# The last stage of an attention and experts kernel takes the tokens without an expert first, and prepares its first group in the experts' last tile

## What is computed

```python
NT, D, E, F = 3072, 512, 8, 1024          # 4 batches x 768 tokens
# experts
do_compute = (x @ w_skip) > 0             # the other tokens keep their x
e_idx = argmax(x @ w_gate)                # one expert for each computed token
gate_w = softmax(x @ w_gate)[e_idx]
x[mask] = x[mask] + gate_w * (relu(x[mask] @ w1[e]) @ w2[e])   # w1[e] 512x1024, w2[e] 1024x512
# last stage
h = maximum(maximum(x @ w1, x @ w2), x @ w3)                   # 512x768 each
out = h @ w_out                                                # 768x512
```

## Time and profile before

| | us |
|---|---|
| median of 3 runs | 704.7 (704.05 to 705.7) |
| profiled execution | 703.12, its span 701.3 |
| PE busy | 663.9 (95%) |
| DVE busy | 468.5 (67%) |
| ACT busy | 326.8 (47%) |
| POOL busy | 125.6 (18%) |
| mean granted clock of PE | 0.985 of full speed |

### The profile page before, as it was taken

One profiled execution on the slowest core, in us unless ns is written; L12 is line 12 of the kernel. 1 busy time (PEld: TensorE's weight loads), 2 busy tenths in 40 slices (PEclk: granted clock), 3 DMA queues, 4 the chain that ended last, 5 costly groups with the idle time before them and its releaser, 6 DMA issues.

```text
span 701.3 us, 13203 instructions
## 1 busy us (share of the span) xinstructions
PE 663.9 (95%) x4903; PEld 555.2 (79%) x4903; DVE 468.5 (67%) x811; ACT 326.8 (47%) x509; POOL 125.6 (18%) x153
## 2 busy tenths in 40 slices
PE   4999965999999999996899999999999999999998
PEld 3778852899999999984688888878888887888886
DVE  4778867666567656757898886258878625887510
ACT  3445422555555555545455645244554525455321
POOL 7321122425444545440000000000000000000000
PEclk9999986999999999999999999999999999999999
DMA  8999954655765565566111111511111111110011
GB/s 301 411 335 325 363 193 176 231 196 194 236 221 194 184 229 202 189 219 233 37 60 61 60 36 71 179 46 61 60 62 32 73 61 45 61 61 30 1 54 67
DMA packets 34548, 102.57 MB, mean 146 GB/s; under 512 B 5644, under 2 KB 5772, under 8 KB 34384
## 3 DMA queue, kind: packets, MB, share of 16 engines
q1 hardware_dynamic: 30640, 96.04, 39.2%
q0 software_dynamic: 3296, 5.00, 2.0%
q10 hardware_dynamic: 576, 1.05, 0.4%
HBM read 89.20 MB, written 16.79 MB: 151 GB/s over the span
## 4 chain that ended last, share of the span: by engine, by line
PE 52%; DMA 2%; DVE 2%; ACT 1%; issue 1%; POOL 0%; SPq 0%; DVEq 0%; POOLq 0%; ACTq 0%
PE ps_c L1333 8%; PE ps_c L1334 8%; PE ps_c L1335 8%; PE ps_b L1333 5%; PE ps_b L1335 5%; PE ps_b L1334 5%; PE ps_f L1334 2%; PE ps_f L1333 2%; PE ps_f L1335 2%; PE ps_a L1333 2%; PE ps_a L1335 2%; PE ps_a L1334 2%; DMA x_in<-x_dram,idx_g 1%; DMA f_in<-x_dram 1%; PE ps_a L1395 0%
## 5 line engine op out<-in xcount | busy, mean ns | idle before, releaser
L991 DVE TENSOR_TENSOR w_lo<-raw,w_hi 128x1024 fp32r<-128x1024 f32 x66 | 82.4, 1258 | 52.6 <-ACT w_hi L650 52.6
L650 ACT ACTIVATE w_hi<-raw 128x1024 fp32r<-128x1024 f32 x67 | 71.0, 1059 | 61.1 <-PE ps_y L1335 50.5
L1333 PE MATMUL ps_c<-c_hi,u_lo 128*128 128x512 f32 x216 | 85.8, 397 | 4.9 <-DVE c_lo L1061 2.9
L1014 DVE TENSOR_TENSOR u_lo<-u_f,u_hi 128x1792 fp32r<-128x1792 f32 x27 | 54.7, 2025 | 52.0 <-ACT u_hi L640 48.1
L1334 PE MATMUL ps_c<-c_lo,u_hi 128*128 128x512 f32 x216 | 84.2, 390 | 0.0
L1335 PE MATMUL ps_c<-c_hi,u_hi 128*128 128x512 f32 x216 | 84.1, 389 | 0.0
L1333 PE MATMUL ps_h<-x_hi,w_lo 128*128 128x256 f32 x256 | 72.3, 283 | 0.6 <-DVE x_lo L998 0.3
L1335 PE MATMUL ps_h<-x_hi,w_hi 128*128 128x256 f32 x256 | 72.4, 283 | 0.0
L1334 PE MATMUL ps_h<-x_lo,w_hi 128*128 128x256 f32 x256 | 72.4, 283 | 0.0
L609 ACT ACTIVATE f_u<-ps_c 128x512 f32<-128x512 f32 x58 | 34.7, 598 | 67.5 <-PE ps_c L1335 65.2
L640 ACT ACTIVATE u_hi<-u_f 128x1792 fp32r<-128x1792 f32 x27 | 46.0, 1702 | 29.4 <-PE ps_c L1335 27.6
(11 more groups left out here) (217 smaller groups left out, 1453.4 us busy)
## 6 DMA issues: line engine op xcount, KB each, us to landing
raw<-wpack SPq DMA_DIRECT2D x67, 512.0 KB, 3.9
u_f<-wunit SPq DMA_DIRECT2D x27, 512.0 KB, 3.3
v_sb<-vW SPq DMA_DIRECT2D x32, 390.0 KB, 5.7
k_sb<-kT SPq DMA_DIRECT2D x32, 250.0 KB, 5.1
q_sb<-qT SPq DMA_DIRECT2D x16, 384.0 KB, 6.1
x_dram<-x_buf SPq DMA_DIRECT2D x4, 1536.0 KB, 10.5
out<-f_out SPq DMA_DIRECT2D x24, 256.0 KB, 2.0
f_in<-x_dram SPq DMA_DIRECT2D x2, 2048.0 KB, 9.1
```

The costliest lines, as they stand in the source:

```text
L650: act.activation(w_hi[c % RING][:, :], raw[:, c % RAW, :], ACT.Copy).then_inc(s_whi, 1)
L991: dve.tensor_tensor(w_lo[c % RING][:, :], raw[:, c % RAW, :], w_hi[c % RING][:, :].bitcast(F32), ALU.subtract).then_inc(s_wlo, 1)
L1014: dve.tensor_tensor(u_lo[n % UBUF][:, 1:8, :], u_f[n % UBUF][:, 1:8, :], u_hi[n % 2][:, :, :].bitcast(F32), ALU.subtract).then_inc(s_ulo, 1)
L1333: pe.matmul(out_, a_lo, b_hi, start=first, stop=False, skip_group_check=goes_on)
```

## The change

**Order of tokens.** The last stage takes its 3072 tokens in an order of its own: first those without an expert, then the rest. DVE works out each token's place from the ranks (a ninth column in the one-hot rows counts the tokens without an expert). POOL writes the token numbers to these places in a new DRAM tensor `order_dram`, by 24 indirect DMAs of one column each: 12 between the gathers and the scatter of tile 0, 12 at the same point of tile 1; behind tile 1's scatter it loads the list into `order`. All loads of x rows for the last stage (eight indirect gathers for each group) and all stores to `out` (24 indirect scatters) go by this list, on POOL instead of SP and ACT.

**First group in the experts' last tile.** The first 1024 tokens of that order have no expert (if there are fewer, two empty tiles are added). POOL gathers them in the last but one tile, behind that tile's gathers and ahead of its scatter. The last tile stands outside the loop: PE turns their rows in two halves (slots 0 and 5), ACT and DVE make the splits of the first half between their old steps and those of the second half behind the tile. The last tile gathers no next x and loads no next weights. The keep-warm matmuls, `first_rows`, `first_unit`, `first_sums` and the wait of PE for the last scatter ahead of unit 0 are gone.

**Layout.** SBUF tensors are placed so that f_in, c_hi, c_lo and the first units' buffers share no space with what the experts' last tile still uses; PSUM banks a, b, c, f are in another order, and group 0 is turned into other banks than the groups behind it. The raw unit 1 is loaded at the start of the experts, unit 2 at their end, `wout` after the last scatter.

The diff, cut to its core:

```diff
+MINT = 5
+SPARE = 2
+TILES = NT // TOK + E - 1 + SPARE
...
 # SP
+            load_unit(1)
...
-            with sp.Fori(0, count) as i:
+            with sp.Fori(0, rest + 1) as i:
...
+            sp.wait_ge(s_landed, rest + 3)
             sp.dma_start(o_f[:, :, :], wout).then_inc(s_oload, 16)
...
 # POOL
+            def put_rows(i, more):
                 pool.tensor_copy(idx_s[:, :], idx[:, bass.ds(i * TB, TB)]).then_inc(s_idxs, 1)
...
+            def list_tokens(t0, t1):
+                for t in range(t0, t1):
+                    pool.indirect_dma_start(
+                        out=order_dram[:, :], out_offset=bass.IndirectOffsetOnAxis(ap=place[:, t:t + 1], axis=0),
+                        in_=token[:, t:t + 1], in_offset=None,
+                        bounds_check=bound, oob_is_err=False).then_inc(s_listed, 16)
+
+            def load_rows(g, signal):
+                for t in range(TG):
+                    at = g * TG + t
+                    pool.indirect_dma_start(
+                        out=f_in[:, t, :], out_offset=None, in_=x_dram[:, :],
+                        in_offset=bass.IndirectOffsetOnAxis(ap=order[:, at:at + 1], axis=0),
+                        bounds_check=bound, oob_is_err=False).then_inc(signal, 16)
+
+            take_rows(0)
+            next_rows(0)
+            pool.wait_ge(s_place, 1)
+            list_tokens(0, NTT // 2)
+            put_rows(0, True)
+            take_rows(1)
+            next_rows(1)
+            list_tokens(NTT // 2, NTT)
+            put_rows(1, True)
+            pool.wait_ge(s_listed, 16 * NTT)
+            pool.dma_start(order[:, :], order_dram.rearrange("(p t) o -> p (t o)", p=P)).then_inc(s_order, 16)
+            with pool.Fori(2, rest) as i:
+                take_rows(i)
+                next_rows(i)
+                put_rows(i, True)
+            i = rest
+            take_rows(i)
+            next_rows(i)
+            pool.wait_ge(s_order, 16)
+            load_rows(0, s_fin)
+            pool.wait_ge(s_fin, 16 * TG)
+            put_rows(i, True)
+            i = rest + 1
+            take_rows(i)
+            put_rows(i, False)
...
+            pool.wait_ge(s_ftr, 2)
+            load_rows(1, s_fin)
+            for g in range(NG):
+                for t in range(TG):
+                    if t == TG // 2 and g + 2 < NG:
+                        pool.wait_ge(s_ftr, 2 * g + 4)
+                        load_rows(g + 2, s_fin)
+                    store_rows(g, t)
...
 # ACT
+            last = rest + 1
+            for f in range(FB):
+                hidden_high(last, f)
+                if f + LEAD < FB:
+                    split_w(last, f + LEAD)
+                if f == 1:
+                    turned_21_22(0, 0)
+                    turned_11_12(0, 0)
+                if f == 2:
+                    sum_1(0, 0)
+                if f == 3:
+                    sums_2_3(0, 0)
+                if f == 4:
+                    sum_4(0, 0)
+                if f == 6:
+                    turned_21_22(0, 1)
+                    turned_11_12(0, 1)
+            unit_high(1)
+            sum_1(0, 1)
+            sums_2_3(0, 1)
+            sum_4(0, 1)
...
 # DVE
+            step(dve.scalar_tensor_tensor(out=behind_skip[:, :], in0=token_f[:, :], scalar=total[:, E:E1], in1=skips,
+                                          op0=ALU.add, op1=ALU.subtract))
...
+            dve.scalar_tensor_tensor(out=place[:, :], in0=place_row[:, :], scalar=float(NTT), in1=place_blk[:, :],
+                                     op0=ALU.mult, op1=ALU.add).then_inc(s_place, 1)
...
+            last = rest + 1
+            for f in range(FB):
+                hidden_low(last, f)
+                if f == 0:
+                    split_w(last, LEAD - 1)
+                if f + LEAD < FB:
+                    split_w(last, f + LEAD)
+                if f == 0:
+                    unit_low(0)
+                if f == 1:
+                    sum_1(0, 0)
+                if f == 2:
+                    sums_2_3(0, 0)
+                if f == 3:
+                    low_11_sum_4(0, 0)
+                if f == 4:
+                    low_12(0, 0)
+                if f == 5:
+                    low_sums_1_2(0, 0)
+                    unit_sums(1)
+                if f == 6:
+                    low_sums_3_4(0, 0)
+            sum_1(0, 1)
+            sums_2_3(0, 1)
+            low_11_sum_4(0, 1)
+            low_12(0, 1)
+            low_sums_1_2(0, 1)
+            sums_out(last)
+            low_sums_3_4(0, 1)
+            dve.wait_ge(s_landed, rest + 3)
...
 # PE
+            last_tile = rest + 1
+            first_product(last_tile, 0)
+            for f in range(FB):
+                if f + 1 < FB:
+                    first_product(last_tile, f + 1)
+                if f == 0:
+                    turn_rows(0, 0)
+                    pe.wait_ge(s_xo, last_tile * TB + TB)
+                if f == 5:
+                    turn_rows(0, 1)
+                second_product(last_tile, f)
```

More of the change, by code:

```diff
@@ L128, in build @@
         g_in = sb("g_in", [P, TB])
+        g_nat = sb("g_nat", [P, TB])
+        idx_g = sb("idx_g", [P, TB], I32)
+        idx_s = sb("idx_s", [P, TB], I32)
+        idx_q = sb("idx_q", [P, TB], I32)
+        token = sb("token", [P, NTT], I32)
+        token_f = sb("token_f", [P, NTT])
+        place = sb("place", [P, NTT], I32)
+        order = sb("order", [P, NTT], I32)
+        gate = sb("gate", [P, NTT])
         with ExitStack() as att:
@@ L471, in _ @@
                         load_unit(n + UBUF)
-                for t in range(TG):
-                    if t == TG // 2 and g + 2 < NG:
-                        load_rows(g + 2)
-                    store(g, t)
             for i in range(OUTS):
@@ L537, in _ @@
             pool.wait_ge(s_table, 1)
-            count = pool.value_load(table[0:1, MAXT + 1:MAXT + 2], min_val=1, max_val=MAXT)
+            rest = pool.value_load(table[0:1, TILES:TILES + 1], min_val=MINT - 2, max_val=TILES - 2)
             bound = pool.to_reg(NT - 1)
@@ L565, in _, with take_rows @@
             gather_gates()
-            with pool.Fori(0, count) as i:
+            def take_rows(i):
                 for t in range(TB):
@@ L642, in _ @@
             act.wait_ge(s_table, 1)
-            count = act.value_load(table[0:1, MAXT + 1:MAXT + 2], min_val=1, max_val=MAXT)
+            rest = act.value_load(table[0:1, TILES:TILES + 1], min_val=MINT - 2, max_val=TILES - 2)
             act.sem_inc(s_used, RING)
@@ L672, in _ @@
                         split_w(i + 1, f + LEAD - FB)
-            act.wait_ge(s_landed, count + 1)
-            act.sem_inc(s_pass, 1)
-            act.wait_ge(s_wlo, count * FB + RAW + LEAD - 1)
-            for t in range(1, TG, 2):
-                act.dma_start(f_in[:, t, :], x_f[0][:, t, :]).then_inc(s_first[t], 16)
             def high(c, k, x):
@@ L1357, in _ @@
             keep_warm(ps_y[0], ones[:, :], oh_row[:, 0:DM // P, :].rearrange("p t r -> p (t r)"), 5)
-            with pe.Fori(0, count) as i:
+            with pe.Fori(0, rest + 1) as i:
                 first_product(i, 0)
```

458 lines of the change are left out of this document (220 added, 238 removed).

## The result

The changed kernel takes 724.5 us (median; 723.7 to 725.1) against 705.2 for the kernel before: 1.0275 times its time, 95% interval 1.0255 to 1.0295. The forecast was 720.9 with a range of 709 to 731, and 0.89 on slower. The profiled execution of the changed kernel took 725.0 us, with a span of 723.2 against 701.3, so the traces differ by 21.9 us.

The account below looks back on a forecast made before the run. PE, busy 95% of the span, was taken as the bound, with POOL's chain feeding it x. Terms 0.4 + 17.0 + 1.5 - 4.4 + 1.5 + 0.2 = +16.2 us gave 720.9 us, range 709 to 731.

Parts of the forecast that it names:

- Routing: Between attention and the first tile: more and wider DVE operations cost 0.4 us (0 to 0.8); `place` operations are covered.
- The list: Tiles 0 and 1: 24 one-column scatters on POOL, 1.41 us each, make PE 17.0 us late by tile 2.
- The landing: Tile 2's x: second gather issued at 202.4 lands 5.1 us later, at 207.5 (landings 3.7 to 7.1 us).
- The clock: Behind PE's long waits in tile 2 and the last tile: half speed for 3 us costs 1.5 us each.
- The last tile: Experts' last tile: PE waits 7.9 us (5.8 to 10.9) for gathered f_in; experts end at 324.0 instead of 312.02.
- The seam: Between experts and last stage: unit 1 starts at 336.0 against 340.38, a gain of 4.4 us (9 to 0).
- The change of groups: Last stage, group 0: `load_rows(2)` ahead of stores 4 to 7 delays ACT and PE 1.5 us (0.5 to 3.5).
- The end: End of the program: the last store, now a scatter on POOL, costs 0.2 us (0 to 1).
- The first (a covered list): Tiles 0 and 1: list scatters at 0.8 us or less fit POOL's idle time; -2.3 us, 702.4; chance 0.07.
- The second (rows in time): Last tile: first group's x is there by 290.4, seam closed in full; +6.8 us, 711.5; chance 0.08.
- The fourth: POOL's queue backs up everywhere: 1.55 us a step, 7.1 to landing, 3.5 in the rows; +26.9, 731.6; chance 0.15.
- The fifth: PE's clock holds in both waits: 717.9 us, inside the forecast's own range; no separate chance given.

Follow-up runs that it names:

- The kernel kept warm: Against the changed kernel: 40 keep-warm matmuls put ahead of PE's turning of group 0's tokens in the experts' last tile; 725.53 us, ratio 1.0293 to the kernel before.
- The kernel with the loads moved: Against the changed kernel: group 2's rows loaded behind all eight stores of group 0 instead of ahead of stores 4 to 7; 722.75 us, ratio 1.0238.

## Why the prediction was right

The path that it named is the path that the trace shows: the list fills POOL's queue, the scatter and the next gather come late, and PE waits for x in tiles 1 and 2, then for the first group's rows. Two terms were clearly off in size, the landing and the change of groups, and one, the end, was put at next to nothing.

*Routing:* forecast 0.4, measured 1.1. PE turns its first x 0.1 us later (119.76 against 119.65), but the next 1.08 (144.29 against 143.21), with a wait of 1.31 us for DVE's w_lo between them in place of 0.28. The cover for the seven operations for `place` held: DVE splits the first x at 122.08, before at 122.04. What took longer is the next split, 2.42 us in place of 1.39. POOL's copy to `x_nat` now starts inside it, at 123.58 in place of 122.50, since the gates come later. That this meeting is the reason is read from the times; no run takes it away.

*The list:* right. From the gates' end to the scatter tile 0 took 19.3 us, forecast 17.9; the steps came 1.46 us apart there and 1.38 in tile 1, forecast 1.41. The place of each scatter was forecast within 2 us (153.7 and 189.3; measured 155.6 and 189.7), POOL's way to tile 2's second gather within 0.9 (202.4; 201.48).

*The landing:* here the term was mis-sized. The sum let PE wait for the second gather and 5.1 us of landing, 207.5; it started at 203.66. PE turns the first half when the first gather is in, issued at 200.12: 3.5 us. Of the 3.8 us, 1.4 come from the first gather in place of the second, 1.6 from the landing and 0.9 from POOL. The view of x_in gives 3.5, 4.1 and 4.8 us (least, middle, most) between 165 and 206, where the earlier trace rows gave 3.7, 5.1 and 7.1. The queues were emptier: DMA share 0.31 there, 0.65 to 0.74 in the stretches before PE's turns in the kernel before. The weights' loads wait for `w_lo`, and that stops when PE does. So PE is 13.6 us late at tile 2's turn, where the forecast had 17.4 (0.4 and 17.0), by the forecast's own mechanism. The Trainium skill gives 2.0 us plus the bytes over 436 GB/s, 2.6 us for 256 KB (DMA: Bandwidth & Descriptors, Anatomy of one DMA — SWDGE (gpsimd) path). The changed kernel's second trace has one such landing, at this place, while all other gathers of x_in in the two traces took 2.9 us or more. As an estimate by that page PE would have started at 202.7.

*The clock:* behind tile 2's wait it cost 1.9 us, forecast 1.5; the kernel kept warm gives 2.0 for the one in the last tile, counted from the landing. It also fell behind tile 1's wait of 2.3 us (tile 1 took 1.7 us longer without its waits), which cost nothing: POOL set the time of the next turn, and PE waited so much less.

*The last tile:* forecast 7.9 us of wait, measured 10.2. The eighth gather starts 12.0 us behind the first in place of 9.9: two of them took 1.92 and 2.77 us, beside DVE's splits, which the change itself makes more. The forecast knew the price of such a meeting from the earlier trace rows, but only as one end of its range (1.55 us a step). The landing was 5.4, forecast 5.1.

*The seam:* forecast -4.4, measured -3.2. From the landing to the experts' end it was 25.5 us against 25.7, and unit 1 starts 11.0 us behind that, against 12.0; the 2.3 us of the wait are what is missing.

*The change of groups:* forecast 1.5, measured 3.8, beyond the 3.5 given as its upper bound. Store 4 is issued at 465.48; less the 12.2 us of lateness there it is 453.3, forecast 452.5. PE is 2.1 us late behind it, still near the forecast; what was missed is the clock's fall behind PE's wait, 1.7 more. The kernel with the loads moved gives 3.7 for the whole. This part is partly chance: in three of the eight traces with that wait the clock held, and the term was 2.1.

*The end:* forecast 0.2 (0 to 1), measured 5.85. The step that failed is "the last store": it was sized by the landing of a scatter, and what counts is what comes behind the last indirect DMA of POOL. The kernel before had its last one in the last tile of the experts, so its trace could not show it. What POOL or the chip does in that time isn't shown by any run.

The sum, term by term: 16.2 - 3.8 (tile 2's turn) + 0.4 (clock) + 1.2 (last tile and seam) + 2.3 (groups) + 5.65 (end) = 21.95, and the traces have 21.9. By the medians the change costs 19.3. The forecast came within 3.6 us of the median partly by luck: a term 3.8 us too large and one of 5.65 that was missing have opposite signs.

*The rivals.* The first (a covered list) would have needed 0.8 us a step; they took 0.98 at least, with 0.30 between. The second (rows in time) fell at 10.2 us. The third needed both. The fourth, a queue that backs up everywhere, did not come: where PE waited the landings got shorter, and only its 3.5 us for the rows were reached, by POOL's order and the clock. The fifth fell: the clock was at 0.50 behind both waits.

## What to carry to other kernels

An engine with a low busy share can still be full in one place: read its idle time per stage of the loop, and count the new steps against that. Here a tile behind the first held four steps; two rows of 12 cost 14 us that the same steps spread over five tiles did not. When work goes to POOL's queue, look at what is last on it in each stage, the end of the program included.

## What the runs showed of the hardware

- The span ended 5.6 to 7.1 us behind POOL's last indirect DMA in each of the eleven traces where that DMA ended less than 3 us before ACT's last copy, or after it: 7.1 in five traces of kernels with the list in two tiles, 6.1 in three with it in four, 5.6 in three with it in five. Where the last two stores or all of them were plain DMAs (three traces), it ended 2.5 to 2.8 us behind ACT's last copy. Why it goes by the kernel isn't known.
- An indirect DMA of 128 rows takes POOL 0.98 us at the least and 0.30 between two, whether a row is 4 bytes or 2 KB. Of all in the 14 traces three in five took at most 1.02; the longest, 2.77, ran beside DVE's splits.
- Behind a wait of PE of 2.18 to 2.23 us at the same place of the program, the granted clock fell in five traces and held in three. The fall cost 1.6 us. Behind the waits of 7 to 10.5 us in tile 2 and the last tile it was at 0.50 and cost 1.4 to 2.9 us.
- ACT's pauses without a releaser in the core (up to 6.0 us, and one of DVE of 2.0) came in the four traces from one chip and in none of the ten others.
